# A recurrence and two expert layers on one core: routing by gathers, logits made on the way

## The chip, the cores and the metric

The kernel runs on one core of one Trainium2 chip. The metric is the device time of one execution in microseconds (us); several runs of a kernel are compared by their median.

## The reference, cut to what matters

```
# attention-like recurrence, batch 4, 8 heads, 768 steps, head size 40
y[t]  = r[t] @ state
Sa    = state @ a[t]
state = state * w[t] - outer(Sa, b[t]) + outer(v[t], k[t])
x = y as rows: N = 3072 tokens, D = 320
# expert layer 0: E = 8, F = 1024
e = argmax(x @ w_gate);  gate = softmax(x @ w_gate)[e]
out0 = gate * sigmoid(x @ w_output_gate)[e] * (relu(x @ w1[e]) @ w2[e])
# expert layer 1: the same on out0, without the output gate, and each
# expert takes its first `capacity` = 768 tokens; others give 0
```

All data are float32. Each token goes through one expert per layer.

## The kernel before, in words

**Recurrence.** The steps are cut into 12 sets (NK = 12) of two batches and 128 steps, each set into two chunks of 64. A loop over slots j = -3 .. 12 is written out, and in it each engine has its own part, in an order written by hand: SyncE loads inputs and passes small matrices through memory for another layout, TensorE makes the products, VectorE solves triangular blocks and masks, ACT copies products out of PSUM, GpSimd scales. At the end of a set `turn_y(k)` turns the result into rows on TensorE (eight transposes), and `x_out(k)` copies them on ACT into `x_all`, which holds all 3072 rows in SBUF. In slots 0 to 7 SyncE also writes `empty` over a quarter of `x_sorted` of one layer (`clear_sorted`).

**Routing**, once per layer. Six lots of four token tiles: TensorE turns x (L1108), multiplies with the router's weights (L1118) and turns the logits (L1126), with copies on ACT and VectorE between. Then some 35 small VectorE operations in a row, each linked to the one before by a semaphore: argmax as one-hot, softmax gate, position of each token in its expert (counts come from two TensorE products, L1133), number of tiles per expert (at most MT = 31 in all, each of 128 places), and the slot of each token. GpSimd then scatters the rows with gate and token number into `x_sorted` in memory, 24 indirect DMAs of 128 rows (L606). In layer 1 the rows are read back into `x_all` first.

**Expert tiles**, 31 per layer, in loops of two tiles per turn on every engine. TensorE's order is `up(i+1)` (L1156, L1163), `turn_x(i+2)` (L1143), `down(i)` (L1175); ACT copies x turned (`x_turned`), applies half of the relu (`relu0`) and issues the load of the next tile's rows (`load_rows`, L778); VectorE copies the tile's w1 from the ring of two experts to `w1_now` (`stage_w1`, L1424), does the other half of the relu (`relu1`, L1431), reads the token numbers (L1447) and scales the result (`result`, L1439); GpSimd loads a tile's gate and token numbers (`load_meta`, L613) and scatters the result rows (`send`, L620). SyncE loads an expert's weights (`load_expert`, L507 and L510) when the last tile of the expert two before it is done, and the first two after the recurrence's last copy:

```
sp.wait_ge(x_copied, 2 * NK)
...
load_expert(0, 0)
load_expert(0, 1)
```

Of the kernel before, what the change touches and what calls it, by code (L numbers as in the profile page):

```python
# [36 lines left out]
P = 128  # L37
# [5 lines left out]
SIDE = (0, 64)  # L43
NT = S // P
# [6 lines left out]
ROW = DM + 2  # L51
NO_TOKEN = 4096
LOT = 4
E = 8
F = 1024
# [8 lines left out]
TABLES_IN = 16 * 8  # L64
STEP_EXP, STEP_ONEHOT, STEP_SIG = 3, 7, 9
# [6 lines left out]
CLEAR_PARTS = 4  # L72
# [7 lines left out]
    "later": C,  # L80
    "solve_init": BLK * BLK,
# [4 lines left out]
    "tile_rows": N // P,  # L86
    "alternate": E - 1,
    "token_no": NG,
# [3 lines left out]
def tables():  # L92
    import numpy as np

    t = {n: np.zeros((P, w), np.float32) for n, w in TABLES.items()}
    t["ident"] = np.eye(P, dtype=np.float32)
    d = np.arange(D)
    t["eyes"][d, d] = 1
    t["eyes"][64 + d, d] = 1
    j, i = np.arange(P)[:, None], np.arange(P)[None, :]  # L100
# [7 lines left out]
    t["tile_rows"][:] = P * np.arange(N // P)  # L108
    t["token_no"][:] = row[:, None] + P * np.arange(NG)
    t["alternate"][:] = (-1.0) ** np.arange(E - 1)  # L110
    return np.concatenate([t[n] for n in TABLES], axis=1)


def recurrence_and_experts(nc, aT, bT, kT, wT, rT, vT, vN, table, cap, router_w, w1, w2, out):

    with ExitStack() as ctx:
# [38 lines left out]
        eyes = tab("eyes")  # L155
        solve_init = tab("solve_init", BLK, BLK)


        abk_in = sb("abk_in", [P, 5, 2, NPAIR, P])
# [31 lines left out]
        x_all = sb("x_all", [P, NG, ROW])  # L191


        wr = [sb(f"router{s}", [P, 3, 2 * E]) for s in range(2)]
# [9 lines left out]
        slot_i = sb("slot_i", [P, NG], U32)  # L204
# [14 lines left out]
        ring1 = part(AG[:, :, :, :, :, :].rearrange("p u o b a t -> p (u o b a t)"), 0, 2, W1_COLS)  # L219
        ring2 = part(abk_in[:, :, :, :, :].rearrange("p n b a t -> p (n b a t)"), 0, 2, FC, DM)  # L220
        w1_now = part(rvm[:, :, :, :, :].rearrange("p n b a t -> p (n b a t)"), 0, 2, W1_COLS)

        onehot, scratch, expo, counts, upto, rank = (part(G_flat, n * NG * E, NG, E) for n in range(6))
        above = part(G_flat, 6 * NG * E, E, N // P)
        logits = part(G_flat, 7 * NG * E, NG, 2 * E)
        past = part(G_flat, 9 * NG * E, MT, E - 1)
        xT_route = [[F_flat[:, (n * 3 + k) * 512:(n * 3 + k + 1) * 512] for k in range(3)] for n in range(2)]
        logitsT = [F_flat[:, (6 + n) * 512:(7 + n) * 512] for n in range(2)]

        x_rows = y_flat[:, 0:DM]  # L230
        y_rows = y_flat[:, DM:2 * DM]
        xT = part(y_flat, 2 * DM, 3, P)
        hidT = [part(H_flat, n * F, FC, P) for n in range(2)]
        empty = sb("empty", [P, ROW])
        meta = sb("meta", [P, 2])
        token_i = sb("token_i", [P, 1], U32)
# [3 lines left out]
        x_sorted = [nc.dram_tensor(f"x_sorted{s}", [MT * P, ROW], F32, kind="Internal").ap()  # L240
                    for s in range(2)]
        between = nc.dram_tensor("between", [N, DM], F32, kind="Internal").ap()
# [61 lines left out]
        empty_set = sem("empty_set")  # L304
        numbered = sem("numbered")
        sorted_cleared = sem("sorted_cleared")
        w_landed = sem("w_landed")

        def layer_sems(*names):
# [3 lines left out]
            "rt_ready", "rt_copied", "logit_ready", "route_step", "expo_done", "sig_done",  # L313
            "count_ready", "routed", "scattered", "x_landed", "xt_ready", "xt_copied", "w1_ready",
            "h_ready", "h_relu_act", "h_relu_dve", "o_ready", "o_copied",
            "o_stored", "meta_landed", "sent", "meta_ready", "lt_ready", "lt_copied")
        lot_landed = [sem(f"lot_landed_{n}") for n in range(NG // LOT)]

# [38 lines left out]
        def _(sp):  # L357
            sp.dma_start(table_sb[:, :], table).then_inc(tables_in, 16)
            sp.dma_start(cap_i[:, :], cap).then_inc(tables_in, 16)
            for s in range(2):  # L360
                for k, (at, w) in enumerate(KCH):
                    sp.dma_start(wr[s][0:w, k, :], router_w[s, at:at + w, :]).then_inc(tables_in, 16)
# [71 lines left out]
            def clear_sorted(n):  # L434
                s, m = divmod(n, CLEAR_PARTS)
                rows = slice(m * 8 * P, min((m + 1) * 8, MT) * P)
                tiles = (rows.stop - rows.start) // P
                sp.dma_start(x_sorted[s][rows, :].rearrange("(i p) r -> p i r", p=P),
                             empty[:, :].unsqueeze(1).to_broadcast([P, tiles, ROW])
                             ).then_inc(sorted_cleared, 16)  # L440

            for j in SLOTS:
# [49 lines left out]
                if j == 0:  # L492
                    sp.wait_ge(empty_set, 2)
                if 0 <= j < 2 * CLEAR_PARTS:
                    clear_sorted(j)

            sp.wait_ge(x_copied, 2 * NK)

            def load_expert(s, e):

                q = s * E + e
                sp.wait_ge(w_landed, 16 * WEIGHT_DMAS * q)
                at = 0
                for rows, cols in W1_PARTS:
                    w = cols[1] - cols[0]
                    q = slice(64, P) if rows[0] == 2 * P else slice(0, rows[1] - rows[0])
                    sp.dma_start(ring1[q, e % 2, at:at + w], w1[s, e, rows[0]:rows[1], cols[0]:cols[1]]  # L507
                                 ).then_inc(w_landed, 16)
                    at += w if rows[1] - rows[0] == P else 0
                sp.dma_start(ring2[:, e % 2, :, :],  # L510
                             w2[s, e].rearrange("(k p) d -> p k d", p=P)).then_inc(w_landed, 16)

            load_expert(0, 0)
            load_expert(0, 1)


            for q in range(2, 2 * E):
                s, e = divmod(q, E)
                s0, e0 = divmod(q - 2, E)
                if e == 0:  # L520
                    sp.wait_ge(L["routed"][0], 1)
                if e == 2 or q == 2:
                    sp.wait_ge(L["routed"][s], 1)
# [8 lines left out]
            sp.wait_ge(L["o_stored"][1], 16 * MT)  # L532
# [3 lines left out]
        def _(pool):  # L536
            for t in (abk_in, T_T, S_nat):
                nc.gpsimd.memset(t[:, :], 0.0).then_inc(cleared, 1)
            nc.gpsimd.memset(empty[:, 0:DM + 1], 0.0).then_inc(empty_set, 1)
            nc.gpsimd.memset(empty[:, DM + 1:ROW], float(NO_TOKEN)).then_inc(empty_set, 1)  # L540
            pool.wait_ge(tables_in, TABLES_IN)
            nc.gpsimd.tensor_copy(x_all[:, :, DM + 1:ROW], tab("token_no").unsqueeze(2)
                                  ).then_inc(numbered, 1)
            pool.wait_ge(cleared, CLEARS)
            pool.wait_ge(numbered, 1)
# [53 lines left out]
            for s in range(2):  # L599

                pool.wait_ge(L["routed"][s], 1)
                if s == 0:
                    pool.wait_ge(x_copied, 2 * NK)
                    pool.wait_ge(sorted_cleared, 16 * 2 * CLEAR_PARTS)
                for t in range(NG):
                    pool.indirect_dma_start(  # L606
                        out=x_sorted[s],
                        out_offset=bass.IndirectOffsetOnAxis(ap=slot_i[:, t:t + 1], axis=0),
                        in_=x_all[:, t, :], in_offset=None).then_inc(L["scattered"][s], 16)
# [900 lines left out]
```

## Time and profile before

| | before |
|---|---|
| median of 3 runs | 1363.74 us (1363.5 to 1364.49) |
| profiled execution: time, span | 1370.99 us, 1369.1 us |
| TensorE: matmul busy, instructions | 1079.5 us (79%), 19760 |
| TensorE: weight loads, instructions | 915.0 us (67%), 19761 |
| VectorE, ACT, GpSimd busy | 471.5, 262.4, 353.6 us |
| mean granted TensorE clock | 0.85 of full speed |
| shares of the chain: TensorE, "issue", GpSimd, VectorE, DMA | 74%, 9%, 5%, 5%, 4% |

The chain is followed back from the last instruction; at each step it goes to what released it. "issue" is time for which the profile shows no releaser. A float32 product stands in the profile as two records, a transpose as one.

### The profile page before, as it was taken

What the parts mean: (1) busy time and instruction counts of PE and PEld (TensorE: products, weight loads), DVE (VectorE), ACT (ScalarE), POOL (GpSimd) and SP (SyncE); (2) the same over time, 40 slices, a digit from 0 to 9 for tenths busy, and PEclk for the clock granted to TensorE, in tenths of its full rate; (3) what the DMA queues carried; (4) which work ended last, traced back from release to release, by engine and by line L of the source; (5) the groups of instructions that cost most, each with busy time, mean ns of one, the idle gap of its engine ahead of it and who ended that gap; (6) DMA issues with size and microseconds to landing.
All of it is one profiled execution on the core that took longest, in us unless ns stands there. A gap on an engine that the chain in (4) does not pass through costs nothing.

```text
span 1369.1 us, 45453 instructions
## 1 busy us (share of the span) xinstructions
PE 1079.5 (79%) x19760; PEld 915.0 (67%) x19761; DVE 471.5 (34%) x891; ACT 262.4 (19%) x524; POOL 353.6 (26%) x302
## 2 busy tenths in 40 slices
PE   1287777887887888850999999997713999998996
PEld 1277777777787777620888888885303888886884
DVE  7554434534455332250223233231140232322321
ACT  0143333433333333210111011110100110100100
POOL 4443043313444210007112212121034122111211
PEclk8577787787877877885899999999856999999998
DMA  2344543435444221223133333332412313344110
GB/s 80 90 104 114 119 115 93 128 108 122 111 100 125 66 44 48 79 81 116 30 107 109 105 110 109 107 115 61 136 46 85 103 40 110 113 125 157 33 29 1
DMA packets 158724, 125.79 MB, mean 92 GB/s; under 512 B 91498, under 2 KB 136046, under 8 KB 158576
## 3 DMA queue, kind: packets, MB, share of 16 engines
q1 hardware_dynamic: 139216, 93.56, 25.0%
q10 hardware_dynamic: 12096, 14.09, 3.5%
q0 software_dynamic: 7264, 15.86, 3.4%
q8 instruction: 129, 2.11, 0.7%
q14 instruction: 19, 0.16, 0.0%
HBM read 89.60 MB, written 36.16 MB: 92 GB/s over the span
## 4 chain that ended last, share of the span: by engine, by line
PE 74%; issue 9%; POOL 5%; DVE 5%; DMA 4%; ACT 2%; SPq 1%; POOLq 0%; ACTq 0%; DVEq 0%
PE pair L1175 18%; PE pair L1156 16%; PE pair L1163 5%; POOL x_sorted L606 4%; PE bank L1026 3%; PE bank L939 2%; PE pair L1118 2%; PE pair L845 2%; PE pair L1143 2%; PE pair L862 2%; PE bank L1034 2%; PE pair L908 2%; PE pair L879 2%; PE pair L1008 2%; PE pair L894 2%
## 5 line engine op out<-in xcount | busy, mean ns | idle before, releaser
L1175 PE MATMUL pair<-abk_in,H_nat 128*128 x992 | 279.1, 434 | 1.8 <-DVE y_T L1439 1.7
L1156 PEld LDWEIGHTS pair<-y_T,rvm 128*128 128x128 f32 x1984 | 238.1, 197 | 19.7 <-issue 7.2
L1156 PE MATMUL pair<-y_T,rvm 128*128 128x128 f32 x1984 | 239.4, 281 | 8.6 <-DVE rvm L1424 6.3
L1175 PEld LDWEIGHTS pair<-abk_in,H_nat 128*128 128x128 f32 x992 | 183.7, 190 | 72.9 <-issue 3.0
L792 ACT ACTIVATE H_nat<-pair 128x512 f32<-128x512 f32 x62 | 37.0, 597 | 527.0 <-PE pair L1163 527.0
L1424 DVE COPY rvm<-AG 128x2560 f32 x62 | 97.1, 1567 | 96.4 <-issue 74.6
L1143 PE MATMUL pair<-table_sb,y_T 128*128 128x128 f32 x186 | 34.6, 296 | 92.9 <-DMA y_T<-x_sorted 92.9
L554 POOL TENSOR_TENSOR AG<-abk_in,F_run 40x512 f32<-40x512 f32 x48 | 60.4, 1259 | 175.5 <-DVE T_nat L1257 156.1
L568 POOL TENSOR_SCALAR_AFFINE_SELECT AG<-AG 64x512 f32<-64x512 f32 x48 | 54.9, 1145 | 179.7 <-ACT AG L647 177.3
L1431 DVE TENSOR_SCALAR H_nat<-pair 128x512 f32<-128x512 f32 x62 | 42.7, 688 | 147.8 <-PE pair L1163 147.8
L606 POOL DMA_INDIRECT x_sorted<-x_all,slot_i x48 | 50.5, 1053 | 146.8 <-DVE x_all L1415 132.8
L1143 PEld LDWEIGHTS pair<-table_sb,y_T 128*128 128x128 f32 x186 | 19.6, 143 | 101.1 <-issue 93.8
L620 POOL DMA_INDIRECT out<-y_T,token_i x31 | 42.6, 1374 | 171.4 <-DVE y_T L1439 160.3
L620 POOL DMA_INDIRECT between<-y_T,token_i x31 | 45.5, 1468 | 153.7 <-DVE y_T L1439 153.7
L613 POOL DMA_DIRECT2D meta<-x_sorted x62 | 35.6, 574 | 177.2 <-DMA between<-y_T,token_i 90.4
L1163 PE MATMUL pair<-y_T,rvm 64*128 64x128 f32 x992 | 72.0, 285 | 0.0
L1447 DVE CAST token_i<-meta 128x1 uint32<-128x1 f32 x62 | 9.5, 153 | 176.2 <-DMA meta<-x_sorted 176.2
L1163 PEld LDWEIGHTS pair<-y_T,rvm 64*128 64x128 f32 x992 | 60.2, 187 | 7.5
L1439 DVE TENSOR_SCALAR y_T<-pair,meta 128x320 f32<-128x320 f32 x62 | 34.2, 551 | 86.0 <-PE pair L1175 83.9
L561 POOL TENSOR_TENSOR abk_in<-abk_in,E_run 128x1024 f32<-128x1024 f32 x24 | 56.0, 2335 | 1.9
L1274 DVE TENSOR_TENSOR y_T<-bank,F_run 128x512 f32<-128x512 f32 x24 | 16.6, 690 | 115.8 <-PE pair L1044 81.0
L647 ACT ACTIVATE y_T<-pair 128x384 f32<-128x384 f32 x62 | 30.1, 486 | 98.4 <-PE pair L1143 98.4
(140 smaller groups left out, 1498.8 us busy)
## 6 DMA issues: line engine op xcount, KB each, us to landing
abk_in<-w SPq DMA_DIRECT2D x16, 1280.0 KB, 8.5
y_T<-x_sorted ACTq DMA_DIRECT2D x62, 160.0 KB, 2.3
AG<-w SPq DMA_DIRECT2D x16, 512.0 KB, 3.6
AG<-w SPq DMA_DIRECT2D x32, 256.0 KB, 4.5
x_sorted<-empty SPq DMA_DIRECT2D x6, 1288.0 KB, 8.1
t_dram<-T_rows SPq DMA_DIRECT2D x12, 384.0 KB, 2.5
AG<-w SPq DMA_DIRECT2D x32, 128.0 KB, 5.0
w_in<-wT SPq DMA_DIRECT2D x48, 80.0 KB
```

Source lines behind the costliest of these rows:

```text
L554: nc.gpsimd.tensor_tensor(heads(AG[q, u % 5, o]), heads(a_in[q, :, :, c * C:(c + 1) * C]), fruns(k)[q, c::CC, 0:C], ALU.mult).then_inc(a_s ...
L561: nc.gpsimd.tensor_tensor(runs, runs, E_run[:, k % 2, 2:].rearrange("p (n t) -> p n t", t=C + 1)[:, :, 0:C], ALU.mult).then_inc(signal, 1)
L568: return nc.gpsimd.affine_select(t, t, [[0, t.shape[1]], [1, C]], ALU.is_gt, 0.0, base=0, channel_multiplier=-1)
L606: pool.indirect_dma_start(out=x_sorted[s], out_offset=bass.IndirectOffsetOnAxis(ap=slot_i[:, t:t + 1], axis=0), in_=x_all[:, t, :], in_off ...
L620: pool.indirect_dma_start(out=result_of[s], out_offset=bass.IndirectOffsetOnAxis(ap=token_i[:, 0:1], axis=0), in_=y_rows[:, :], in_offset= ...
L1026: mm(bank[6][head_rows(o), at:at + C], S_nat[:, u % 2, o, b, a, :], r_in[k % 2][:, b, a, c * C:(c + 1) * C], start=(a == 0 and b == 0), st ...
L1143: last = nc.tensor.transpose(view(4, 3, P)[:, k, :], x_rows[:, at:at + P], ident)
L1156: mm(to, w1_now[:, par, k * F + m * P:k * F + m * P + P], xT[:, (0, 2 - m // 4)[k], :], start=(m % 4 == 0 and k == 0), stop=False, skip_gr ...
L1163: last = mm(view(2 * par + half, 4, P)[:, m, :], w1_now[q, par, at:at + P], xT[q, 1 + half, :], start=False, stop=True, skip_group_check=True)
L1175: last = mm(bank[5][:, 0:DM], hidT[par][:, k, :], ring2[:, bass.ds(place, 1), k, :].rearrange("p a d -> p (a d)"), start=(k == 0), stop=(k ...
L1424: v.tensor_copy(w1_now[:, par, :], ring1[:, bass.ds(place, 1), :].rearrange("p a f -> p (a f)")).then_inc(L["w1_ready"][s], 1)
L1431: v.tensor_scalar(hidT[par][:, 4:8, :], view(2 * par + 1, 4, P), 0.0, None, ALU.max).then_inc(L["h_relu_dve"][s], 1)
```

## The change

- Logits are made in the recurrence: `turn_y` becomes an ordinary product with a matrix that holds the identity and, beside it, the router's rows of each head, so that 16 partial logits per token come out with the rows. ACT copies them (`lg_parts`), VectorE adds the four parts (`lg_sum`).
- `x_all` goes. ACT copies the rows to `x_stage` and writes them to `x_dram` by two DMAs per set on its own queue (`write_x`). `x_sorted`, its clears, the meta loads and the turning of x for the router go.
- For layer 1, VectorE makes each tile's logits from its result rows (`next_logits`: a product over 8 x 320 elements and a sum), they are sent as eight more columns of `between`, and one DMA on GpSimd's queue reads all of them back.
- The routing sorts token numbers and gates by 24 products on TensorE of one-hot matrices that VectorE makes (`in_place`, `in_tile`, `carried`), and six products that feed nothing (`WARM`) stand ahead of them. `token_all` and `gate_all` then hold both for each place of each tile; x rows are gathered by indirect DMA from `x_dram` or `between`, three tiles ahead (`AHEAD`) into three buffers. Results go out of two buffers.
- w1 is copied by ACT in place of VectorE. The ring for w1 has memory of its own, and the first expert is loaded before the recurrence is over. The tile loops are written out.

```diff
 def x_out(k):                                  # ACT
     act.wait_ge(x_ready, k + 1)
+    if k >= 2:
+        act.wait_ge(x_written[k % 2], 32 * (k // 2))
...
-        copy(x_all[:, (2 * s + b) * NT + t, 0:DM]..., pair[2]..., x_copied)
+        copy(x_stage[:, k % 2, b, :]..., pair[2]..., x_copied)
+    copy(lg_parts[:, 2 * s * NT + t:(2 * s + 1) * NT + t + 1:NT],
+         pair[2][:, :, :].rearrange("p b (a t) -> p b a t", t=P)[:, :, :, D:D + 2 * E], x_copied)
+def write_x(k):
+    act.wait_ge(x_copied, 3 * (k + 1))
+    t, s = set_of(k)
+    for b in range(2):
+        at = ((2 * s + b) * NT + t) * P
+        act.dma_start(x_dram[at:at + P, :], x_stage[:, k % 2, b, :]).then_inc(x_written[k % 2], 16)
+def turn_router():
+    act.dma_start(wr_dram, router_w[1, :, 0:E].rearrange("d e -> e d"), ...).then_inc(wr_turned, 16)
...
-        last = nc.tensor.transpose(pair[2][:, b, a * P:(a + 1) * P], y_T[:, b, a, :], ident)
+        last = mm(pair[2][:, b, a * P:a * P + SPAN], y_T[:, b, a, :], turns[:, a, :], start=True, stop=True)
...
+def lg_sum(k):                                 # VectorE
+    t, s = set_of(k)
+    dve.wait_ge(x_copied, 3 * (k + 1))
+    here = slice(2 * s * NT + t, (2 * s + 1) * NT + t + 1, NT)
+    v.tensor_reduce(lg_all[:, here, :], lg_parts[:, here].rearrange("p g a x -> p g x a"),
+                    AX_X, ALU.add).then_inc(lg_summed, 1)
...
-sp.wait_ge(x_copied, 2 * NK)                   # SyncE
+sp.wait_ge(nat_ready, NU)
+sp.wait_ge(gk_ready, NU)
+sp.wait_ge(r_ready, NU)
 load_expert(0, 0)
+sp.wait_ge(y_ready, NU)
 load_expert(0, 1)
+sp.wait_ge(wr_turned, 16)
+sp.dma_start(wr_next, wr_dram.unsqueeze(0).to_broadcast([P, E, DM])).then_inc(wr_landed, 16)
...
+for n in range(WARM):                          # TensorE, routing
+    mm(bank[7], ident, table_sb[:, 0:512], start=True, stop=True)
+for g in range(NG):
+    if g % (NG // PARTS) == 0:
+        pe.wait_ge(L["place_set"][s], g // (NG // PARTS) + 1)
+    last = mm(bank[6][:, 0:2 * MT], in_place[:, g, :], carried[:, g, :, :]..., start=(g == 0), stop=(g == NG - 1))
...
+def gather(i):                                 # GpSimd
+    if i >= AHEAD:
+        pool.wait_ge(L["xt_ready"][s], i - AHEAD + 1)
+    pool.indirect_dma_start(out=x_rows[i % AHEAD][:, 0:(DM, ROW)[s]], in_=source_of[s],
+        in_offset=...token_all[:, s, i:i + 1]..., bounds_check=last_token, ...).then_inc(x_landed[s][i % AHEAD], 16)
 def send(i):
     pool.wait_ge(L["o_copied"][s], i + 1)
+    if s == 0:
+        pool.wait_ge(lg_made, i + 1)
...
+for i in range(AHEAD):
+    gather(i)
+for i in range(MT):
+    if i + AHEAD < MT:
+        gather(i + AHEAD)
+    send(i)
...
+def next_logits(i):                            # VectorE, layer 0
+    dve.wait_ge(L["o_copied"][s], i + 1)
+    if i:
+        dve.wait_ge(lg_made, i)
+    v.tensor_tensor(terms, wr_next[:, :, :],
+                    y_rows[i % 2][:, 0:DM].unsqueeze(1).to_broadcast([P, E, DM]), ALU.mult).then_inc(terms_made, 1)
+    dve.wait_ge(terms_made, i + 1)
+    v.tensor_reduce(y_rows[i % 2][:, DM:ROW], terms, AX_X, ALU.add).then_inc(lg_made, 1)
...
+for i in range(MT):                            # ACT; before it stage_w1(0..2), x_turned(0..1), relu0(0)
+    if i + 1 < MT:
+        relu0(i + 1, (i + 1) % 2)
+    if i + 2 < MT:
+        x_turned(i + 2)
+    if i + 3 < MT:
+        stage_w1(i + 3, (i + 3) % 2)
```

VectorE, the later half of the routing of layer 0 before the change, from the row that sums the slots to its end:

```order
L1332 TENSOR_REDUCE best<-G_b 128x24
L1404 CAST slot_i<-best 128x24
L1406 TENSOR_TENSOR G_b<-table_sb,tile_end 128x217
L1409 TENSOR_REDUCE tile_f<-G_b 128x31
L1410 TENSOR_TENSOR G_b<-G_b,table_sb 128x217
L1412 TENSOR_REDUCE tile_f<-G_b 128x31
L1413 CAST tile_i<-tile_f 128x62
L1415 COPY x_all<-gate 128x24
```

and the same place after the change:

```order
L1332 TENSOR_REDUCE best<-G_b 128x24
L1394 CAST place_i<-best 128x24
L1395 TENSOR_SCALAR row_i<-place_i 128x24
L1396 TENSOR_SCALAR place_i<-place_i 128x24
L1397 TENSOR_TENSOR F_run<-table_sb,place_i 128x744
L1400 TENSOR_TENSOR T_T<-F_run,table_sb 128x24x31
L1402 TENSOR_TENSOR T_T<-F_run,gate 128x24x31
L1406 TENSOR_TENSOR F_run<-table_sb,row_i 128x768 x4
L1412 TENSOR_TENSOR G_b<-table_sb,tile_end 128x217
```

Between the slot and the tile table (G_b<-table_sb,tile_end) stand seven more wide operations than before.

GpSimd, at the turn from layer 0 to layer 1 before the change (a loop's last tile, then the routing's scatters):

```order
L620 DMA between<-y_T,token_i 3072x320
L606 DMA x_sorted<-x_all,slot_i 3968x322 x24
L613 DMA meta<-x_sorted 128x2
L620 DMA out<-y_T,token_i 3072x320
L613 DMA meta<-x_sorted 128x2
```

and after the change:

```order
L627 DMA y_T<-x_dram,token_all 128x320
L637 DMA between<-S_nat,token_all 3072x328 x4
L616 DMA lg_all<-between 128x24x8
L627 DMA y_T<-between,token_all 128x328 x4
L637 DMA out<-S_nat,token_all 3072x320
```

The 24 scatters are gone, the logits' load stands alone between the last store and the first gather, and there is no meta load between stores.

ACT, the first tiles of layer 0 after the change (H_nat from a 128x384 view is x turned, rvm<-ring_own is the copy of w1; before, rows L792, L647 and a DMA L778 repeat, without a copy of w1):

```order
L656 ACTIVATE rvm<-ring_own 128x2560
L808 ACTIVATE H_nat<-pair 128x512
L656 ACTIVATE H_nat<-pair 128x384
L813 TENSOR_LOAD tile_i
L813 ISA x2
L813 TENSOR_LOAD tile_i
L813 ISA x2
L815 ISA
L656 ISA
L656 ACTIVATE rvm<-ring_own 128x2560
```

The copy of w1 for a later tile now stands in ACT's row between one tile's turned x and the next tile's relu.

## Rows read from the trace of the kernel before

**Rows 1.** Windows, layer 0's tiles: start:end, length, busy us (instructions) per engine
```profile
652.30:945.00 292.70, 292.10 (x2058) 245.43 (x2058) 86.41 (x119) 30.07 (x61) 60.15 (x58) 0.99 0.31 93
```
**Rows 2.** The chain between the recurrence and layer 0: start us, us, what
```profile
570.64 1.97 PE pair L1108 x16
...
600.43 0.36 DVE best L1350
...
613.26 0.20 DVE x_all L1415
...
613.75 1.16 POOL x_sorted L606
...
645.55 2.79 DMA x_sorted<-x_all,slot_i
648.36 2.32 DMA y_T<-x_sorted
...
652.27 2.93 PE pair L1156 x12
```
**Rows 3.** The same chain between the layers
```profile
945.05 0.56 DVE y_T L1439
...
955.01 5.90 DMA between<-y_T,token_i
...
997.58 0.36 DVE best L1350
...
1011.16 0.20 DVE x_all L1415
...
1049.53 5.56 PE pair L1156 x32
```
**Rows 4.** The same chain at the first wait for weights, layer 1
```profile
1230.77 8.25 DMA abk_in<-w
...
1239.15 1.50 DVE rvm L1424
```
**Rows 5.** Groups by line and shape; GpSimd's from the page
```profile
L1431 DVE TENSOR_SCALAR H_nat<-pair 128x512 f32<-128x512 f32 x62 | 42.7, 688 | 147.8 <-PE pair L1163 147.8
...
L1280 DVE TENSOR_TENSOR rvm<-pair,table_sb 128x1024 f32<-128x1024 f32 x24 | 29.4, 1223 | 14.6 <-PE pair L1012 13.6
...
L1254 DVE TENSOR_REDUCE T_rows<-products 128x15 f32<-128x225 f32 x12 | 4.7, 390 | 0.4
...
L647 ACT ACTIVATE U_T<-pair 128x512 f32<-128x512 f32 x24 | 14.3, 597 | 0.6
...
L647 ACT ACTIVATE G_b<-pair 128x1024 f32<-128x1024 f32 x12 | 12.3, 1024 | 37.9 <-PE pair L826 37.9
...
L613 POOL DMA_DIRECT2D meta<-x_sorted x62 | 35.6, 574 | 177.2 <-DMA between<-y_T,token_i 90.4
```
**Rows 6.** TensorE's timeline: turn_y at two clocks, and the up projection
```profile
236.17 1.09 PE L1044 MATMUL pair<-table_sb,y_T 128*128 128x128 f32 x8
...
323.00 1.97 PE L1044 MATMUL pair<-table_sb,y_T 128*128 128x128 f32 x8
...
1304.40 3.73 PE L1156 MATMUL pair<-y_T,rvm 128*128 128x128 f32 x32
```
**Rows 7.** Gaps on the chain, first and last of eight, one without clear, a clear
```profile
117.19 2.94 issue
...
413.86 4.28 issue
...
457.03 1.48 issue
...
413.09 0.41 SPq L438 DMA_DIRECT2D x_sorted<-empty  x1
```
**Rows 8.** DMA: GpSimd's queue in 945:965, and all meta loads
```profile
q0 software_dynamic: 128, 0.00, 1.2%
...
meta<-x_sorted POOLq DMA_DIRECT2D x62, 1.0 KB, 2.0
```

More of the change, by code:

```diff
@@ L50 @@
 DM = H * D
-ROW = DM + 2
 NO_TOKEN = 4096
-LOT = 4
+PARTS = 4
 E = 8
+ROW = DM + E
 F = 1024
@@ L99, in tables @@
     t["eyes"][64 + d, d] = 1
+    for at in range(NPAIR):
+        t["turns"][d, at * SPAN + d] = 1
+        t["turns"][64 + d, at * SPAN + 64 + d] = 1
     j, i = np.arange(P)[:, None], np.arange(P)[None, :]
@@ L190, in recurrence_and_experts @@
         y_T = sb("y_T", [P, 2, NPAIR, P])
-        x_all = sb("x_all", [P, NG, ROW])
-        wr = [sb(f"router{s}", [P, 3, 2 * E]) for s in range(2)]
+        x_stage = sb("x_stage", [P, 2, 2, DM])
+        lg_all = sb("lg_all", [P, NG, 2 * E])
+        lg_parts = sb("lg_parts", [P, NG, NPAIR, 2 * E])
         cap_i = sb("cap_i", [P, 2], I32)
@@ L432, in fetch_d, with load_expert @@
                                      ).then_inc(d_landed, 16)
[L434 to L440, printed above, removed]
+            def load_expert(s, e):
+                q = s * E + e
+                sp.wait_ge(w_landed, 16 * WEIGHT_DMAS * q)
+                at = 0
+                for rows, cols in W1_PARTS:
+                    w = cols[1] - cols[0]
+                    q = slice(64, P) if rows[0] == 2 * P else slice(0, rows[1] - rows[0])
+                    sp.dma_start(ring1[q, e % 2, at:at + w], w1[s, e, rows[0]:rows[1], cols[0]:cols[1]]
+                                 ).then_inc(w_landed, 16)
+                    at += w if rows[1] - rows[0] == P else 0
+                sp.dma_start(ring2[:, e % 2],
+                             w2[s, e].rearrange("(k p) d -> p k d", p=P)).then_inc(w_landed, 16)
             for j in SLOTS:
@@ L1182, in _ @@
                 turn_x(1)
-                def tile(i, par, up_next=True, turn_next=True):
-                    if up_next:
-                        up(i + 1, 1 - par)
-                    if turn_next:
+                for i in range(MT):
+                    if i + 1 < MT:
+                        up(i + 1, (i + 1) % 2)
+                    if i + 2 < MT:
                         turn_x(i + 2)
-                    down(i, par)
-                tile(0, 0)
-                with pe.Fori(1, (MT - 1) // 2) as j:
-                    tile(j * 2 - 1, 1)
-                    tile(j * 2, 0)
-                tile(MT - 2, 1, True, False)
-                tile(MT - 1, 0, False, False)
+                    down(i, i % 2)
         @block.vector
@@ L1470 @@
+                if s == 0:
+                    dve.wait_ge(wr_landed, 16)
+                relu1(0, 0)
+                for i in range(MT):
+                    if i + 1 < MT:
+                        relu1(i + 1, (i + 1) % 2)
+                    result(i)
+                    if s == 0:
+                        next_logits(i)
 def kernel(**inputs):
```

399 lines of the change are left out of this document (170 added, 229 removed).

## The prediction

> **What bounds the kernel now.** I read the windows first, to see which engine is full in which stage, then the chain that ended last, stage by stage, and then single lines for prices. In the first expert layer TensorE is busy for 292.1 of 292.7 us [rows 1]: 31 tiles of 128 tokens, 9.45 us each, and nothing else can be gained inside it. The expert layers are therefore the fixed part, and the question is what stands between them. The chain shows two long stretches in which the expert matmuls wait:
>
> - Between the recurrence and the first up projection, 570.64 to 652.27, 81.6 us [rows 2]: 29.8 us of transposes and router matmuls until the first reduction of the routing (600.43), 13.0 us of small VectorE operations, each waiting for the one before (to 613.46), then 24 scatters on GpSimd, one after another, up to 645.55, their landing, one load of x rows, one turn of x.
> - Between the layers, from the end of the down projection of tile 29 (945.02) to 1049.53, 104.5 us [rows 3]: the last result waits for the tile before it to be stored and for its meta row, the store, the load of all of x, the same transposes (the routing's first reduction is at 997.58), the same routing, the same scatters.
>
> Two smaller things: in the second layer an expert with one tile makes TensorE wait for weights, twice [rows 4], and in the recurrence TensorE has gaps that no semaphore explains ("issue"), the longest just behind a clear of x_sorted [rows 7].
>
> **The change, part by part.** *Routing of layer 0.* The transposes and router matmuls go away, since logits come with turn_y. From the instant at which the last two x copies end (570.64 now) the new path is: 0.4 us because turn_y is longer (below), 0.3 for the third ACT copy of 128 columns, 0.3 for the last lg_sum, then the routing chain. Its present 13.0 us lose the copy of counts (0.4), eight scans of 0.24 each (1.9), and the casts and copies that leave it (0.6); they gain one scan over 192 (0.4, taken like the other 192-wide operations), three 24-wide operations (0.6), one 744-wide comparison and two 744-wide products, four 768-wide comparisons, and two final conversions (0.4). A wide operation is priced from two rows [rows 5]: 390 ns at 225 elements and 1223 ns at 1024 give 1.04 ns per element, so 0.93 us at 744 and 0.96 at 768. That is 2.8 and 3.8 us. The chain becomes 13.0 - 2.9 + 8.0 = 18.1, say 18.3 us with the waits. The 24 sorting matmuls run beside the comparisons and the four operations on past behind them (1.6 us), so I cost them at nothing; without that cover they are 24 times about 0.2, 5 us. The six warming matmuls lie between the counts and the first comparison (about 10 us of VectorE work), where TensorE has nothing else. Then a gather: 0.3 until GpSimd starts, 1.16 on GpSimd and a landing as for the last scatter, whose 2.79 us run from its start, 3.2 with the longer first issue [rows 2]; then 1.6 for turning x into xT, as now between 650.68 and 652.27. Sum 0.4 + 0.3 + 0.3 + 18.3 + 0.3 + 3.2 + 1.6 = 24.4. **Gain 81.6 - 24.4 = 57 us.** The w1 copy by ACT (2.3 us, below) starts when routing ends and is done before xT.
>
> *Between the layers.* From the end of down of tile 29 on: its result 0.6; next_logits, two operations over 2560 elements, 390 ns + 2335 x 1.04 ns = 2.8 each, 5.7 with the wait, and the result of tile 30 is queued behind them on VectorE (to 6.3, where its down projection is done at 4.9); that result 0.6, its own next_logits 5.7 (12.6); GpSimd's send 0.8, and its landing, which now takes 5.90 us beside the load of expert weights [rows 3], and I take 5 (18.4). Then the load of logits, which the trace of before doesn't have: 3072 pieces of 32 B on GpSimd's queue. The nearest row is meta: 128 packets of 8 B took 1.2% of 16 engines' 20 us, 30 ns each, so 3072 are 5.8 us on 16 engines; a meta load lands in 2.0 us [rows 8], and issuing it costs GpSimd 0.57 us [rows 5]. If that issue doesn't grow with the pieces, the load is 0.6 + 2.0 + 5.8 = 8.4; if it grows with them (24 times 0.57), 21.5. If the transfer were no dearer than meta's, 2.6. I take 10: the issue is mostly a fixed cost in every row here. After it (28.4): the chain 13.8 - 2.9 + 8.1 = 19.0 (before: 997.58 to 1011.36), 0.7 until GpSimd starts, gather 3.2, turn 1.6. Sum 52.9. **Gain 104.5 - 52.9 = 52 us.**
>
> The Trainium skill, DMA: Bandwidth & Descriptors, section "Anatomy of one DMA", says of descriptor generation that "You can emit a lot of descriptors before the incremental cost shows up". By that rule the load of logits would cost 8.4 instead of 10; the 128-row loads here can't show it.
>
> *The tiles.* TensorE has the same work per tile. VectorE's load in layer 0 becomes relu 0.69, result 0.56, next_logits 5.7: 7.0 of 9.45 us, and its 1.6 us copy of w1 is gone. ACT gets that copy: 1024 elements take 1024 ns and 512 take 597 [rows 5], 0.83 ns per element, so 2560 take 2.3 us; ACT is then busy some 3.4 us per tile and 1.2 us more for its register loads. Gathers are issued three tiles ahead, behind sends; a send waits 6.3 us into the next tile and has two tiles until its buffer is needed. All of this is covered by 9.45 us of TensorE; uncovered it costs what is above 9.45, 31 times. What isn't covered are the two weight waits [rows 4]. There the copy follows the landing at once: 2.3 instead of 1.5. And stage_w1(i+2) now stands on ACT ahead of relu0(i+1) and x_turned(i+2), and up(i+2) needs that xT: 0.6 more for the relu (512 elements) and 0.5 for the copy (384, by the same rate). **Loss 2 x 1.9 = 4 us.** No expert of layer 0 has under three tiles.
>
> *The recurrence.* (a) The eight clears of x_sorted, 1.3 MB each, go. Each was followed within 5 us by a TensorE gap without a releaser: 2.94, 2.92, 3.04, 3.60, 3.37, 2.01, 2.10, 4.28 us, mean 3.0; in the same place of the slot without a clear it is 1.48 [rows 7]. Gain 8 x 1.55 = 12 us at most, since other waits can take over. (b) turn_y was a transpose of 128 columns, 1.09 us for eight at the fast clock and 1.97 at the slow one; it becomes an ordinary f32 product over 104 columns. The up projection shows what such a product costs: 32 records, 16 products of 128 columns, in 3.73 us, 233 ns each, so 190 ns at 104 columns and 1.5 us for eight, 3.0 at the slow clock [rows 6]. Loss 0.4 to 1.0 us in each of 12 slots, taken as 6. (c) x rows go to memory on ACT's queue, 0.33 MB a slot, a quarter of a clear, and the third copy is on ACT: 0.3 us ahead of the gk copies. Expert 0's weights (2.6 MB, two clears) are now loaded while the recurrence still runs, where they can hold up two such gaps. I take 6 us for these together, between nothing (the copies and DMA issues on ACT lie in its idle time) and 12. Sum -12 + 6 + 6 = **0**.
>
> Total -57 - 52 + 4 + 0 = -105. The profiled execution's span 1369.1 becomes 1264. It took 1370.99 by the clock outside, and the median of the runs is 7.25 below that; so 1363.74 - 105 = 1259.
>
> **Rivals.** *The first phase keeps its 12 us* (turn_y and ACT's extra work hidden, gaps shorter): for it, TensorE's waits there are nearly all these gaps; against it, slots without a clear are hardly shorter. 1247. *The load of logits is dear*: 21.5, plus a landing of the last store as now; 1272. Nothing in the trace excludes it. *VectorE becomes the bound in layer 0*: it needs over 4.0 us per 2560-wide operation in place of 2.8; the widest VectorE row here (1024) keeps its rate, so it speaks against. At 4.5 each: 1.2 us more for 31 tiles, 1296. *Code streaming, the one that could end on the other side*: the tile loops are written out now, 62 tiles of 133 TensorE instructions (2058 + 2058 in 31 tiles [rows 1]), some 8200, where a loop body of two tiles was reused. If the gaps of the recurrence are fetches of code and one came for every 256 instructions, 32 of them would fall on a saturated TensorE: at 1.48 us 47 us (1306), at the 3.0 beside a large transfer 97, and from 3.3 us each (gain of 105 used up) the kernel is slower; at 4.28, 1396. Against it: in the recurrence 256 instructions pass in 4.7 us (the page's 39521 records less 8246 of the tiles, in 570.6 us), in a tile in 18 us, six times the longest gap seen, so that a fetch ahead has time.
>
> The Trainium skill, Runtime: NRT & Kernel Launch, section "Instruction fetch mechanics", says that code streams in 16 KiB blocks of 256 instructions, the next fetched while one runs, that crossing is mostly hidden, and that a taken branch is what stalls. By that rule writing the loops out costs nothing. The recurrence, which has no branches, doesn't show crossings as hidden (1.48 to 4.28 us).
>
> **How the numbers follow.** Forecast as worked out 0.68 (its own range 1247 to 1272); the recurrence's gain kept, or more, 0.10; dear logits load 0.11; VectorE or another engine over 9.45 in layer 0 0.05; code streaming 0.06, half of it slower than before. The range takes in the first three and a few us on either side for the unknown costs of the recurrence: 1238 to 1284. About 0.2% is what these runs can tell from no change. Faster 0.96, same 0.01, slower 0.03.
>
> **What would show it.** The first up projection some 25 us behind the last x copy, the second layer's some 53 us behind the end of down 29; gathers of 1 us on GpSimd off the chain in the tiles; a tile of 9.45 us in both layers; VectorE 7 us per tile in layer 0; the weight waits some 2 us longer; no 3 us gaps at the places of the clears; turn_y at 1.5 to 3 us. Wrong would be: tiles over 9.45 us, a logits load over 15 us, or a recurrence more than 12 us longer or shorter.

## The result and the profile after

The changed kernel takes 1275.47 us (median of 4 runs, 1268.95 to 1279.12) against 1364.12 us before: a ratio of 0.934, 95% interval 0.931 to 0.938. Forecast were 1259 us, range 1238 to 1284. The time lies in the range; the gain is 89 us where 105 were forecast. From the page of the changed kernel, the span, the busy times, TensorE's granted clock in 40 slices and the shares of the chain:

```profile
span 1272.6 us, 44048 instructions
...
PE 1071.5 (84%) x19712; PEld 931.5 (73%) x19712; DVE 543.1 (43%) x820; ACT 395.4 (31%) x574; POOL 314.8 (25%) x252
...
PEclk9566876787787779787899999999869999998999
...
PE 76%; issue 8%; DVE 7%; DMA 3%; POOL 3%; ACT 2%; SPq 1%; another core or an unknown queue 0%; ACTq 0%; POOLq 0%; DVEq 0%
```

TensorE has nearly its old amount of work (1071.5 us, 1079.5 before); what is gone is waiting. The chain of the changed kernel (start, length, what) has the marks that split the execution into the same stages as [rows 2] and [rows 3]:

```profile
577.36 0.77 ACT x_stage L656 x2
...
578.33 0.38 DVE lg_all L1292
...
592.45 9.79 PE bank L1130 x48
...
603.03 3.17 DMA y_T<-x_dram,token_all
...
607.79 6.67 PE pair L1154 x32
...
895.97 4.52 PE pair L1173 x16
...
910.13 2.83 DVE S_nat L1449
...
913.72 2.39 DMA between<-S_nat,token_all
...
916.39 4.50 DMA lg_all<-between
...
920.92 0.36 DVE best L1339
...
935.92 10.51 PE bank L1130 x48
...
947.21 3.05 DMA y_T<-between,token_all
...
1254.74 4.52 PE pair L1173 x16
...
1260.11 0.98 POOL out L637
```

| stage, us | before | after | difference | forecast |
|---|---|---|---|---|
| recurrence, to the last x copy (570.60; 577.36 + 0.77) | 570.6 | 578.1 | +7.5 | 0 |
| to the first up projection of layer 0 | 81.7 | 29.7 | -52.0 | -57 |
| layer 0, to the end of down 29 (895.97 + 4.52) | 292.8 | 292.7 | 0 | 0 |
| to the first up projection of layer 1 (951.85) | 104.5 | 51.4 | -53.1 | -52 |
| layer 1, to the end of down 29 (1254.74 + 4.52) | 302.1 | 307.4 | +5.3 | +4 |
| from there to the end | 17.5 | 13.3 | -4.1 | 0 |
| sum | 1369.1 | 1272.6 | -96.5 | -105 |

The sum is 96.5 us and not 89, because the profiled execution before took 1370.99 us, 6.9 above the median of its kernel, and the one after 1274.38 us, 1.1 below its own. The tiles have kept their 9.45 us, and the two routings carry the gain. Three rows differ from the forecast by several us: the recurrence, the first routing, and the end.

**The sort shows.** VectorE's timeline in the routing of layer 0 (start, length, operation, in brackets its idle time and the releaser), and last one of its sums in a tile:

```profile
591.44 3.56 DVE L1406 TENSOR_TENSOR F_run<-table_sb,row_i 128x768 f32<-128x768 f32 x4
...
596.17 0.38 DVE L1418 TENSOR_REDUCE tile_f<-G_b 128x31 f32<-128x217 f32 x1
602.34 0.19 DVE L1420 TENSOR_SCALAR token_f<-bank 128x31 f32<-128x31 f32 x1 [5.79 <-PE bank L1130]
...
629.83 2.82 DVE L1449 TENSOR_REDUCE S_nat<-AG 128x8 f32<-128x2560 f32 x1
```

The comparisons are done at 595.00 and the tile tables at 596.55. The prices held: 0.93 us for a 744-wide operation, 0.89 for each of the four comparisons (0.96 forecast), 2.82 for 2560 elements. Then VectorE waits 5.79 us for the last sorting product. TensorE's timeline shows why, below its turn_y at two clocks:

```profile
283.20 2.03 PE L1067 MATMUL pair<-table_sb,y_T 128*128 128x104 f32 x16
...
366.14 3.74 PE L1067 MATMUL pair<-table_sb,y_T 128*128 128x104 f32 x16
...
582.66 7.19 PE L1126 MATMUL bank<-table_sb 128*128 128x512 f32 x12
592.45 9.78 PE L1130 MATMUL bank<-T_T,F_run 128*128 128x62 f32 x48 [2.60 <-DVE F_run L1406]
```

24 products (48 records) take 9.78 us, 0.41 each. In the window 592.0 to 602.4 the granted clock is 0.56 of full speed; over the two turn_y above it is 1.00 and 0.50. My estimate of 0.2 per product was a price for full speed. The six products ahead ended at 589.85 and left a pause of 2.60 us.

**The recurrence has one slot of 60 us.** In each slot SyncE passes the matrix T through memory to change its layout. From one such passing to the next the slots are 31.9, 40.0, 41.5, 41.5, 60.0, 38.5, 40.9, 43.9, 45.4, 42.5, 39.1 us (before: 32.3, 39.6, 45.0, 44.2, 43.1, 45.0, 42.0, 41.3, 44.0, 42.0, 43.0). SyncE's DMA issues of the long one:

```profile
206.95 0.35 SPq L439 DMA_DIRECT2D t_dram<-T_rows  x1
207.35 2.69 SPq L441 DMA_DIRECT2D tn_dram<-T_nat  x1
228.05 4.85 SPq L448 DMA_DIRECT2D T_T<-t_dram  x8
...
266.92 0.36 SPq L439 DMA_DIRECT2D t_dram<-T_rows  x1
```

T is written at 206.95 and fetched again only at 228.05; in the other slots these are 2 to 3 us apart. In 205:230 the queues read (packets, MB, share of 16 engines; q10 is ACT's):

```profile
q10 hardware_dynamic: 1179, 0.00, 30.8%
q1 hardware_dynamic: 952, 0.65, 28.7%
```

1179 packets with almost no bytes hold 31% of the engines' 25 us, 104 ns each. They are `turn_router`, which ACT issues at 197.94: 2560 elements of 4 B. The queue has 6364 packets in the whole execution, and 3796 in the run below that lacks this DMA. Small packets are not always so slow: in the same window of the kernel before, q1 has 6482 packets, most of them under 512 B, at 28 ns each. On the chain, TensorE's products end early in this slot, and it then waits for T:

```profile
219.96 2.64 PE pair L884 x33
...
223.33 4.22 another core or an unknown queue
...
227.57 0.43 ACT ZV L656
```

### The profile page after: what moved, and what is told of

It is laid out like the page before. It is cut to its first block, busy times and chain, and to the rows that moved or that the text cites. A ratio compares the mean times of both kernels' runs of the same rounds, so it can differ in the third digit from the quotient of the medians.

```text
span 1272.6 us, 44048 instructions
## 1 busy us (share of the span) xinstructions
PE 1071.5 (84%) x19712; PEld 931.5 (73%) x19712; DVE 543.1 (43%) x820; ACT 395.4 (31%) x574; POOL 314.8 (25%) x252
## 3 DMA queue, kind: packets, MB, share of 16 engines
q10 hardware_dynamic: 6364, 3.96, 1.9%
## 4 chain that ended last, share of the span: by engine, by line
PE 76%; issue 8%; DVE 7%; DMA 3%; POOL 3%; ACT 2%; SPq 1%; another core or an unknown queue 0%; ACTq 0%; POOLq 0%; DVEq 0%
PE pair L1173 20%; PE pair L1154 18%; PE pair L1161 5%; PE pair L1067 3%; PE bank L961 2%; PE pair L867 2%; PE bank L1048 2%; PE pair L1141 2%; PE pair L884 2%; PE bank L1056 2%; POOL AG L566 2%; PE pair L901 2%; PE pair L916 2%; PE pair L1030 2%; PE bank L1130 2%
## 5 line engine op out<-in xcount | busy, mean ns | idle before, releaser
L1173 PE MATMUL pair<-abk_own,H_nat 128*128 x992 | 277.8, 433 | 1.8 <-DVE S_nat L1438 1.7
L1154 PEld LDWEIGHTS pair<-H_nat,rvm 128*128 128x128 f32 x1984 | 240.3, 199 | 24.2 <-ACT H_nat L656 15.3
L1154 PE MATMUL pair<-H_nat,rvm 128*128 128x128 f32 x1984 | 241.7, 282 | 13.1 <-ACT H_nat L656 13.1
L1173 PEld LDWEIGHTS pair<-abk_own,H_nat 128*128 128x128 f32 x992 | 183.9, 190 | 71.7 <-issue 3.0
L656 ACT ACTIVATE rvm<-ring_own 128x2560 f32 x62 | 145.0, 2339 | 151.3 <-issue 85.2
L1431 DVE TENSOR_SCALAR H_nat<-pair 128x512 f32<-128x512 f32 x62 | 42.6, 686 | 170.2 <-PE pair L1161 170.2
L566 POOL TENSOR_TENSOR AG<-abk_own,F_run 40x512 f32<-40x512 f32 x48 | 60.4, 1258 | 168.9 <-DVE T_nat L1248 149.1
L1445 DVE TENSOR_TENSOR AG<-AG,S_nat 128x2560 f32<-128x2560 f32 x31 | 87.6, 2825 | 1.1
L1449 DVE TENSOR_REDUCE S_nat<-AG 128x8 f32<-128x2560 f32 x31 | 87.4, 2820 | 1.1
L1161 PE MATMUL pair<-H_nat,rvm 64*128 64x128 f32 x992 | 72.1, 285 | 0.0
L1161 PEld LDWEIGHTS pair<-H_nat,rvm 64*128 64x128 f32 x992 | 60.2, 187 | 7.4
L1240 DVE TENSOR_TENSOR products<-T_rows,G_rows 128x1 f32<-128x1 f32 (+4 forms) x180 | 44.5, 247 | 10.5 <-DMA G_rows<-g_dram 4.8
```

The source lines that it names most:

```text
L566: nc.gpsimd.tensor_tensor(heads(AG[q, u % 5, o]), heads(a_in[q, :, :, c * C:(c + 1) * C]), fruns(k)[q, c::CC, 0:C], ALU.mult).then_inc(a_s ...
L656: nc.scalar.activation(dst, src, ACT.Copy, scale=scale).then_inc(signal, 1)
L1154: mm(to, w1_now[:, par, k * F + m * P:k * F + m * P + P], xT[:, (0, 2 - m // 4)[k], :], start=(m % 4 == 0 and k == 0), stop=False, skip_gr ...
L1161: last = mm(view(2 * par + half, 4, P)[:, m, :], w1_now[q, par, at:at + P], xT[q, 1 + half, :], start=False, stop=True, skip_group_check=True)
L1173: last = mm(bank[5][:, 0:DM], hidT[par][:, k, :], ring2[:, bass.ds(place, 1), k, :].rearrange("p a d -> p (a d)"), start=(k == 0), stop=(k ...
L1240: v.tensor_tensor(products[:, 0:t, 0:t], T_rows[:, k % 2, 0:t, BLK:BLK + t], G_rows[:, k % 2, t, 0:t].unsqueeze(1).to_broadcast([P, t, t]) ...
```

## Experiments

All ratios are to the kernel before on the same chip and in the same session, where it had medians of 1373.8 (e1 to e4), 1376.6 (b1, e6 to e8) and 1372.2 us (e9 to e11); stage lengths are from the one profile of each kernel.

### The router's DMA moved to the start

```diff
 load_routers()
+turn_router()
...
-if c == 1 and j == 2:
-    turn_router()
```

> The changed kernel with one move: the DMA that turns the router of layer 1 into wr_dram (2560 elements of 4 B, ACT's queue) is issued at the start, not in slot 2 of the recurrence. Theory A (this DMA holds up the small transfers of the solve: the slot from 206.95 to 266.92 lasted 60 us, its neighbours 41.6 and 38.5): that slot falls to about 42 us, the whole gains 14 to 18 us, 1258 to 1261. Rival B (the long slot is an accident of this execution, or a code fetch): the slot's length doesn't depend on it, 1270 to 1279.

1281.23 us, ratio 0.931 (0.928 to 0.935): no gain that can be told from the changed kernel's 0.934. Yet the long slot is gone (42.5 us in its place); the stall has moved with the DMA. SyncE's issues at the start:

```profile
24.85 6.30 SPq L410 DMA_DIRECT2D w_in<-wT  x4
31.20 16.27 SPq L398 DMA_DIRECT2D abk_own<-aT  x2
...
70.89 0.35 SPq L439 DMA_DIRECT2D t_dram<-T_rows  x1
```

The two loads of a, issued at 31.20, take 16.27 us to issue instead of 0.7, and the first passing of T comes at 70.89 instead of 52.05. So theory A is right that this DMA makes the long slot, and its forecast of the time (14 to 18 us less) failed, because the start isn't a place without small transfers either.

### The sort: no products ahead, or ten

```diff
-WARM = 6
+WARM = 0      # e2
+WARM = 10     # e3
```

> The changed kernel without the six products that feed nothing ahead of the sort (WARM = 0). Theory A (a product after a pause runs at the slow clock, and the six lie too early, 2.6 us before the sort starts, so they do nothing for it): the 24 sorting products take the same 9.8 us (layer 0) and 10.5 us (layer 1), time as after within 2 us. Rival B (they shorten it a little): the sort takes over 10.5 us in layer 0, the whole 1 to 3 us more.

1282.43 us, ratio 0.933 (0.929 to 0.937). TensorE's row in layer 0:

```profile
598.90 10.50 PE L1130 MATMUL bank<-T_T,F_run 128*128 128x62 f32 x48 [9.62 <-DVE F_run L1406]
```

10.50 against 9.78 us, and the same 10.5 in layer 1: the six products were worth 0.7 us in one layer. The other profiles with six give the sort 9.26 to 9.92 us where the pause ahead of it is 2.3 to 2.7 us, and 10.27 to 10.50 where it is 3.3 us or more (layer 0 of e1 among them), as long as with none.

> The changed kernel with ten such products in place of six, so that TensorE is busy until the comparisons are done. Theory A (the pause before the sort costs the clock): the sort starts at full clock and takes about 5 us per layer in place of 9.8 and 10.5, the whole gains 8 to 10 us, and up to 3 more per layer if the first up projection stays fast too. Rival B (the sort is bound by something else than the clock): sort as long as before and starts no earlier, 0 to 2 us slower.

1276.63 us, ratio 0.927 (0.922 to 0.932).

```profile
592.55 9.65 PE L1126 MATMUL bank<-table_sb 128*128 128x512 f32 x20
602.35 5.57 PE L1130 MATMUL bank<-T_T,F_run 128*128 128x62 f32 x48
...
930.19 9.79 PE L1126 MATMUL bank<-table_sb 128*128 128x512 f32 x20
941.25 9.34 PE L1130 MATMUL bank<-T_T,F_run 128*128 128x62 f32 x48 [1.27 <-DVE F_run L1406]
```

In layer 0 the ten end just when the sort begins, and it takes 5.57 us, 0.23 per product. In layer 1 they end 1.27 us too early, and the sort takes 9.34. The granted clock is 1.00 over the first sort and 0.57 over the second, behind ten products of nearly the same length: the clock is the cause, and what differs ahead of the two is the pause. Counted from the two counting products ahead of them, the sort ends 4.2 us earlier than in the changed kernel in layer 0 and 1.2 in layer 1. The whole shows no more than that: its interval overlaps the changed kernel's (0.931 to 0.938), and the 8 to 10 us of theory A did not come. The up projection behind the sort (6.14 us) stayed slow; some 4 us of waiting for gathered rows lie between.

### w1 by VectorE in layer 1

```diff
-                stage_w1(0, 0)                              # ACT; (1, 1) and (2, 0) likewise
+                if s == 0:
+                    stage_w1(0, 0)
...
-                    if i + 3 < MT:
+                    if s == 0 and i + 3 < MT:
                         stage_w1(i + 3, (i + 3) % 2)
...
+                    if s == 1 and i + 2 < MT:               # VectorE, ahead of relu1(i + 1)
+                        stage_on_dve(i + 2)
```

> The changed kernel with w1 copied by VectorE in layer 1 as before the change (ACT still does it in layer 0). Theory A (the two weight waits of layer 1 grew since ACT copies slower, 2.3 for 1.5 us, and reads registers, does the relu and copies xT after it): from the landing to the next up projection 2 us instead of 3.4 per wait, the whole gains 3 to 4 us. Rival B (the landing itself came later): no change beyond 1 us.

1275.09 us, ratio 0.929 (0.925 to 0.934), which by itself can't be told from the changed kernel; layer 1 took 302.9 us from its first up projection to the end of down 29 (302.1 before the change, 307.4 after). The up projections behind the weight waits, with TensorE's idle time in brackets, before the change:

```profile
1240.99 5.39 PE L1156 MATMUL pair<-y_T,rvm 128*128 128x128 f32 x32 [3.29 <-DVE rvm L1424]
...
1264.70 5.44 PE L1156 MATMUL pair<-y_T,rvm 128*128 128x128 f32 x32 [2.99 <-DVE rvm L1424]
```

after it:

```profile
1144.03 6.50 PE L1154 MATMUL pair<-H_nat,rvm 128*128 128x128 f32 x32 [4.82 <-ACT H_nat L656]
...
1171.74 6.31 PE L1154 MATMUL pair<-H_nat,rvm 128*128 128x128 f32 x32 [5.88 <-ACT H_nat L656]
```

and with w1 by VectorE in layer 1:

```profile
1146.02 5.44 PE L1157 MATMUL pair<-H_nat,rvm 128*128 128x128 f32 x32 [4.14 <-issue]
...
1169.92 5.44 PE L1157 MATMUL pair<-H_nat,rvm 128*128 128x128 f32 x32 [3.13 <-issue]
```

6.3 us idle before, 10.7 after, 7.3 here: theory A, 3.4 us. The up projection behind each wait also goes from 5.4 us to 6.5 and 6.3, and back to 5.4 here. The rows correct my prediction too. TensorE idles 3 us per wait; the 8.25 and 1.50 us of [rows 4] run in part while it still works on a tile. The experts there have two tiles, not one. And the copy cost 1.4 us per wait, not 1.9: from the landing of the weights to the up projection it is 3.37 us after and 1.97 before, both times. The rest of the growth in idle time, some 1.5 us, came from the second load, which landed after 9.44 us where it had taken 7.94.

### turn_y alone, in the kernel before

```diff
-last = nc.tensor.transpose(pair[2][:, b, a * P:(a + 1) * P], y_T[:, b, a, :], ident)
+last = mm(pair[2][:, b, a * P:a * P + 104], y_T[:, b, a, :], ident[:, 0:104], start=True, stop=True)
```

> The kernel before with one part of the change: turn_y as an ordinary float32 product over 104 columns (identity) in place of the transpose over 128. Theory A (a float32 product costs about 0.25 us at the fast clock and 0.46 at the slow one whatever its width, as the 16 records in 2.0 and 3.7 us show in the changed kernel): 2.0 to 3.7 us per set in place of 1.1 to 2.0, the recurrence 10 to 18 us longer. Rival B (my prediction's price from the up projection, 1.5 and 3.0 us): 5 to 8 us longer.

1387.26 us, ratio 1.0075 (1.0053 to 1.0096): 10.3 us slower, 7 to 13. Its group (two records per product):

```profile
L1044 PE MATMUL pair<-table_sb,y_T 128*128 128x104 f32 x192 | 35.5, 361 | 3.0 <-issue 2.2 <-DVE y_T L1274 0.8
```

Before, the same line has 96 records and 16.7 us busy: turn_y went from 1.4 to 3.0 us per set, 19 us in all, of which some 10 reached the time. That is the low end of theory A (10 to 18), and the interval touches rival B (5 to 8); the price per set is theory A's. A product over 104 columns takes 0.25 us at the fast clock and 0.47 at the slow one in the rows above (2.03 and 3.74 for eight), not 0.19 and 0.38. The sort's products over 62 columns took 0.23 at the fast clock (e3), and those of the up projection over 128 columns 0.233 [rows 6]: from 62 to 128 columns the width hardly counts, and scaling the price by the columns made it too low.

### The router laid out turned in the input

```diff
-sp.wait_ge(wr_turned, 16)
-sp.dma_start(wr_next, wr_dram.unsqueeze(0).to_broadcast([P, E, DM])).then_inc(wr_landed, 16)
+sp.dma_start(wr_next, router_t.unsqueeze(0).to_broadcast([P, E, DM])).then_inc(wr_landed, 16)
...
-turn_router()
```

> The changed kernel, with the router of layer 1 laid out turned in its input, so that no DMA turns it by 4 B elements. Theory A (that DMA holds up the small transfers wherever it stands: in slot 2 it made a slot of 60 us, at the start it moved the first passing of T from 52 to 71 us): no long slot and no late start, 17 us less, 0.923 of before. Rival B (it only moves other work): a ratio of 0.930 or more.

1266.42 us, ratio 0.921 (0.917 to 0.924), against 0.934 (0.931 to 0.938) with that DMA: 0.0137 of 1364, 19 us (12 to 26), from runs on two chips. Slots of 33.2, 39.7, 41.3, 42.6, 44.6, 40.5, 45.4, 44.0, 43.0, 42.7, 40.8 us, and the first passing of T at 52.14. Theory A, as to there being a cost; its size is less sure. The recurrence ends at 578.1, 584.6, 588.0 and 581.6 us in the four profiles with this DMA in slot 2 (the changed kernel, e2, e3, e4; mean 583.1), and at 572.4 and 575.9 in the two without it (e6, e8): 9 us apart.

### The clears put back

```diff
+if 0 <= j < 8:                                              # SyncE, behind load_bk
+    sp.dma_start(waste[rows, :].rearrange("(i p) r -> p i r", p=P), empty...).then_inc(wasted, 16)
```

> e6 with eight DMAs of 1.3 MB from SBUF to memory that nothing reads, at the places and in the sizes of the clears of before. Theory A (they lengthen the gaps of TensorE that no semaphore explains, 3.0 us for 1.5 each): the recurrence is 8 to 14 us longer than in e6, with gaps of 2 to 4 us behind each. Rival B (other waits take over, since slots without a clear were hardly shorter): 0 to 4 us.

1279.76 us, ratio 0.930 (0.927 to 0.934): 0.0095 above e6, 13 us; the last x copy ends at 581.7 instead of 572.4. Two clears, as SyncE's timeline has them, and the gaps without a releaser that its chain has behind them:

```profile
155.27 0.39 SPq L534 DMA_DIRECT2D waste<-empty  x1
325.71 0.39 SPq L534 DMA_DIRECT2D waste<-empty  x1
```

```profile
159.17 3.37 issue
...
326.22 2.91 issue
```

The time is as theory A has it: the 12 us that the prediction gave for dropping the clears are there. Its mechanism is not shown. Of the eight clears only these two have a gap of over 2 us within 5 us behind them; behind the others it is under 1.8. The longest gap of the run (4.70 us at 228.75) stands 31 us behind a clear, and e6, which has no clears, has one of 3.88 us in the same place (225.43).

### Three mends together

```diff
-for n in range(WARM):
+for n in range((10, 12)[s]):
     mm(bank[7], ident, table_sb[:, 0:512], start=True, stop=True)
...
 last.then_inc(L["sorted_ready"][s], 1)
+for n in range(4):
+    mm(bank[7], ident, table_sb[:, 0:512], start=True, stop=True)
```

with the laid-out router and w1 by VectorE in layer 1.

> e6 with w1 copied by VectorE in layer 1, ten (layer 0) and twelve (layer 1) products that feed nothing ahead of the sort and four behind it. Theory A: the sort takes 5.6 us in both layers (a pause of 1.3 us ahead of it was enough to halve the clock in layer 1 with ten), the first up projection of each layer 3.6 to 4.5 us in place of 6.7 and 5.4, and the weight waits are 1.4 us shorter: 12 to 16 us less than e6, 0.912 of before. Rival B (the pause while the gathered rows are awaited resets the clock anyway): up projections as slow as before, 8 to 11 us less than e6.

1252.21 us, ratio 0.909 (0.906 to 0.912), below e6 by 14 us in the medians and 16 by the ratios. The sort takes 5.47 us in both layers, at a granted clock of 1.00, and the first up projections are fast at once:

```profile
601.83 3.84 PE L1152 MATMUL pair<-H_nat,rvm 128*128 128x128 f32 x32 [0.58 <-ACT H_nat L655]
...
938.63 3.84 PE L1152 MATMUL pair<-H_nat,rvm 128*128 128x128 f32 x32 [0.64 <-ACT H_nat L655]
```

3.84 us each in place of 5.24 and 6.27 in e6 (6.67 and 5.37 in the changed kernel): theory A. This kernel is faster than the one before and than the changed one (0.934).

### The first expert late, and x written twice

```diff
+sp.wait_ge(x_copied, 3 * NK)                                # e9, e11: ahead of load_expert(0, 0)
...
+act.dma_start(x_twice[at:at + P, :], x_stage[:, k % 2, b, :]).then_inc(x_written[k % 2], 16)   # e10
```

> e6 with the first expert's weights loaded after the last x copy, as before the change, not before the recurrence is over. Theory A (the load of 2.6 MB beside the last slots lengthens TensorE's code gaps there: 55.6 us from the last passing of T to the last x copy before the change, 62.5 in e6): the tail gets 1 to 3 us shorter, and the first up projection isn't later, since the weights land 24 us ahead of it or are just in time. Rival B (the tail is longer by its three turn_y and the logits' copy alone): the tail stays within 1 us of e6.

1260.14 us, ratio 0.919 (0.915 to 0.923), e6 had 0.921 (0.917 to 0.924). The tail from the last passing of T to the last x copy is 61.7 us, in e6 62.5. That speaks for rival B, weakly: in the other profiles of kernels that load early the tail is 59.7 to 63.7, so that the 1 to 3 us of theory A would hardly be seen. The profile of b1 shows what rival B says of turn_y: its tail is 60.1, against 55.6 before.

> e6 with every x row written to memory twice (a second buffer that nothing reads), so four DMAs per set on ACT's queue in place of two. Theory A (these writes cost something, ACT's 0.8 us of issues ahead of the copy of Q and 0.33 MB beside the code fetches): the recurrence 3 to 6 us longer than e6. Rival B (they lie in the idle time of ACT and of the DMA engines, as a slot uses 0.35 of them): within 2 us.

1258.64 us, ratio 0.917 (0.915 to 0.920), against 0.921 in e6 on another chip: nothing is lost by writing x twice, rival B.

> e8 (w1 by VectorE in layer 1, products ahead of and behind the sort, laid-out router) with the late first expert of e9. Theory A of e9: 1 to 3 us less than e8, 0.908 of before. Rival B: the same as e8 or, if w1 of expert 0 isn't there in time (10.3 us after its issue, routing takes 25), longer.

1251.34 us, ratio 0.911 (0.908 to 0.914), the same as e8: rival B. The late load now runs beside the first gather, which lands after 4.63 us where it took 3.22 in e8. TensorE's row behind it:

```profile
597.24 0.52 PE L1140 MATMUL pair<-table_sb,y_T 128*128 128x128 f32 x3 [2.08 <-DMA y_T<-x_dram,token_all]
```

The four products behind the sort had ended 2.08 us before it, and yet the granted clock stayed 1.00 and the first up projection took 3.84 us. In e3 a pause of 1.27 us went before a slow sort. So the length of the pause alone does not decide; what does, no run here shows.

## Why the prediction was right, and where its terms were off

The time lies in the stated range (1238 to 1284), but 3.5 us above the narrower one (1247 to 1272) that the prediction gave its own mechanism. The two routings and the tiles came out as it said. That the total came so near is in part luck: errors of opposite sign met between the layers and in the recurrence, where a cost of 9 us or more was missing altogether.

**Routing, layer 0: -52.0 for -57.** The step "The 24 sorting matmuls run beside the comparisons [...] so I cost them at nothing" failed. Its own fallback (24 times 0.2, 5 us) was a price at the fast clock, and the six warming products didn't give that clock. Exposed: 5.8 us. All else is within 1 us: lg_sum, the small operations, gather 3.17 for 3.2, turn of x.

**Between the layers: -53.1 for -52, two errors against each other.** The sort was exposed again (some 6 us). The last store and the load of logits were cheaper: the last store lands 15.6 us after down 29 (18.4 forecast), and the load, in GpSimd's timeline and in the DMA queues of 916.0 to 921.5 (packets, MB, share of 16 engines), takes 4.50 where I took 10:

```profile
916.39 1.48 POOL L616 DMA_DIRECT2D lg_all<-between  x1 [1.70 <-DMA between<-S_nat,token_all]
```

```profile
q0 software_dynamic: 64, 0.10, 15.7%
```

The bound of 21.5 us, an issue growing with the pieces, and the rival built on it (a dear load of logits) are refuted: 24 times the pieces of a meta load cost 1.48 us of issue for 0.57.

**Tiles: as forecast.** 292.70 us for 292.75 in layer 0, VectorE's 2560-wide operations 2.82 us each, so the rival with VectorE as the bound is refuted. Written-out loops cost nothing: the rival of code streaming, the only one that could have ended slower, is refuted by the same number. The Trainium skill (Runtime: NRT & Kernel Launch, "Instruction fetch mechanics") says that crossing a block of code is mostly hidden; in the tiles the trace agrees, since layer 0's differ by 0.05 us over 31 tiles. Whether the gaps of the recurrence are such crossings, no run here shows; without clears they stay, up to 3.88 us in e6.

**Layer 1: +5.3 for +4.** The mechanism stood, with the corrections above: 1.4 us per wait for 1.9, a later landing, and slower up projections behind the longer pauses, which the prediction didn't have. Undoing it gave 3.4 us less idle time and a layer 4.5 us shorter.

**Recurrence: +7.5 for 0.** Of my three terms the clears were sized right (13 us by e7, 12 forecast), though the gaps that were to carry them are not shown there, and turn_y too small (10 by b1, 6 forecast), with the step "so 190 ns at 104 columns" at fault. The third (x writes, third copy, early expert, 6) was nothing for the writes by e10 and nothing measurable for the early load by e9; the third copy was not tested. What the prediction didn't have at all is turn_router: it lists the change's DMAs but not this one, a term put at nothing without a reason, which cost 19 us by the ratios of e6 and 9 by the ends of the recurrence. With the others that is 16 or 6; the profile shows 7.5. Single profiles can't decide it: with the changed kernel's recurrence they end it at 578.1 to 588.0, mean 583.1, which would be +12.5, and the one profile before may itself lie high, since its execution took 6.9 us more than the median. How the rest divides stays open.

**End: -4.1 for 0.** Not priced: the last result no longer waits for the store and the meta row before it.

## What to carry to other kernels

Before a layout is made by DMA, count its elements: 2560 of 4 B cost about as much here (9 to 19 us) as 10 MB of clears (13), and not on their own queue but in small transfers that others wait for, so that moving them didn't help, while laying the data out beforehand did. A float32 product with 128x128 weights took 0.23 to 0.25 us at 62, 104 and 128 columns, so narrow columns didn't make it cheap, and the transpose turned into a product took twice its time. When TensorE is filled with idle products for its clock, let them reach up to the first product that counts: with a pause of 1.27 us behind ten of them the sort was slow (e3), with twelve and no pause it was fast (e8), though a pause of 2.08 us did no harm in e11.

## What I had not expected of the hardware

- Packets of 4 B written to memory held the DMA engines about 104 ns each (1179 in 25 us, 31% of 16 engines), and SyncE's issues on another queue stretched from 0.7 to 16.27 us beside them. The Trainium skill (DMA: Bandwidth & Descriptors, "Specifications") gives 512 B as the least transfer for line rate, with read-modify-write below. The trace agrees that these pieces are dear, but size alone does not give the 104 ns, since other packets, most of them under 512 B, took 28 ns; no run here shows the mechanism.
- 3072 pieces of 32 B, read by one DMA of GpSimd, appear as 64 packets of 1.5 KB and landed in 4.50 us, whereas the 2560 pieces of 4 B on ACT's queue were not combined (2568 packets more than in e6).
- The sort took 0.39 us per product behind a pause of 1.27 us (granted clock 0.57) and 0.23 without one (1.00), behind the same ten products (e3).
